# Local attention inside a fused kernel: one matmul for both heads' scores, one for both heads' values

## What is computed

```python
batch, n_heads, seq, head_dim = 4, 8, 576, 64          # factor = 4
q_d, k_d, v_d = means of q, k, v over groups of 4 positions   # 144 positions
out_d = softmax(q_d @ k_d.T / 8) @ v_d                  # each head
scores = q @ k.T / 8, kept where |i - j| < 4            # local band
out_local = softmax(scores) @ v
x = np.repeat(out_d, 4, axis=2) + out_local             # -> (2304, 512)
h = (x @ w1) * (x @ w2) @ w3;  x = h @ w_out            # d_ff = 1024
h = maximum(maximum(x @ u1, x @ u2), x @ u3);  y = h @ u_out   # d_ff = 768
```

## Time and profile before

| | |
|---|---|
| median of 3 runs | 726.11 us (725.23 to 726.6) |
| profiled execution | 725.54 us, span from first to last instruction 723.8 us |
| PE busy | 713.2 us, 99% |
| PE weight loads (beside matmuls) | 595.1 us, 82% |
| DVE / ACT / POOL busy | 219.8 / 193.0 / 210.9 us |
| granted TensorE clock | 1.00 |

### The profile page before, as it was taken

How to read it: one execution, slowest core, us unless ns; L and a number is a source line. 1 busy time by engine, 2 the same in 40 slices (tenths; PEclk the granted TensorE clock), 3 DMA queues, 4 the chain that set the end, 5 groups by cost and what they waited for, 6 DMA issues and landing times.

```text
span 723.8 us, 14645 instructions
## 1 busy us (share of the span) xinstructions
PE 713.2 (99%) x6560; PEld 595.1 (82%) x6560; DVE 219.8 (30%) x392; ACT 193.0 (27%) x417; POOL 210.9 (29%) x186
## 2 busy tenths in 40 slices
PE   6999999999999999999999999999999999999998
PEld 4778788888888888888888998888888888888898
DVE  3464554414453345411100455111111111111111
ACT  5465423322332233312221533111120112111110
POOL 5799423303232223321220231130122114011210
PEclk9999999999999999999999999999999999999999
DMA  9874122202221121122000320000001000000100
GB/s 321 264 233 142 53 74 74 74 24 75 74 75 54 54 92 58 40 80 81 1 1 0 117 73 1 1 35 24 1 0 60 1 0 25 34 1 1 43 16 29
DMA packets 18590, 43.57 MB, mean 60 GB/s; under 512 B 2144, under 2 KB 2912, under 8 KB 18528
## 3 DMA queue, kind: packets, MB, share of 16 engines
q1 hardware_dynamic: 18528, 42.64, 18.2%
HBM read 37.91 MB, written 4.72 MB: 59 GB/s over the span
## 4 chain that ended last, share of the span: by engine, by line
PE 97%; DMA 1%; POOL 1%; SPq 1%; ACT 0%; DVE 0%; issue 0%
PE psum L346 30%; PE psum L348 29%; PE psum L347 29%; PE psum L385 2%; PE psum L363 2%; PE psum L356 2%; PE psum L394 1%; PE psum L373 1%; DMA attention<-ident 1%; POOL weights_split L738 1%; SPq L310 0%; POOL acts_split L738 0%; ACT attention L622 0%; DVE psum L528 0%; DVE psum L533 0%
## 5 line engine op out<-in xcount | busy, mean ns | idle before, releaser
L346 PE MATMUL psum<-acts_split,weights_split 128*128 128x512 f32 (+1 forms) x992 | 370.3, 373 | 0.6 <-POOL weights_split L738 0.6
L348 PE MATMUL psum<-acts_split,weights_split 128*128 128x512 f32 (+1 forms) x992 | 366.0, 369 | 0.0
L347 PE MATMUL psum<-acts_split,weights_split 128*128 128x512 f32 (+1 forms) x992 | 365.8, 369 | 0.0
L346 PEld LDWEIGHTS psum<-acts_split,weights_split 128*128 128x128 f32 x992 | 187.0, 188 | 34.6 <-issue 2.6
L348 PEld LDWEIGHTS psum<-acts_split,weights_split 128*128 128x128 f32 x992 | 187.0, 189 | 31.7
L347 PEld LDWEIGHTS psum<-acts_split,weights_split 128*128 128x128 f32 x992 | 187.1, 189 | 30.1
L738 POOL TENSOR_TENSOR acts_split<-gate,acts_split 128x512 fp32r<-128x512 f32 (+1 forms) x70 | 82.5, 1179 | 438.0 <-ACT acts_split L622 438.0
L622 ACT ACTIVATE acts_split<-gate 128x512 fp32r<-128x512 f32 (+1 forms) x70 | 41.2, 589 | 246.9 <-DVE gate L608 152.0
L622 ACT ACTIVATE gate<-psum 128x512 f32<-128x512 f32 (+1 forms) x70 | 38.8, 555 | 130.3 <-PE psum L348 130.3
L738 POOL TENSOR_TENSOR acts_split<-xy,acts_split 128x512 fp32r<-128x512 f32 (+1 forms) x44 | 52.2, 1207 | 55.7 <-ACT acts_split L622 55.7
L582 DVE TENSOR_TENSOR gate<-gate,psum 128x512 f32<-128x512 f32 (+1 forms) x40 | 25.4, 634 | 129.0 <-PE psum L348 129.0
(11 more groups left out here) (42 smaller groups left out, 378.4 us busy)
## 6 DMA issues: line engine op xcount, KB each, us to landing
xy<-wa SPq DMA_DIRECT2D x40, 256.0 KB, 5.4
attention<-qk SPq DMA_DIRECT2D x16, 576.0 KB, 4.2
attention<-v_win SPq DMA_DIRECT2D x16, 384.0 KB, 3.4
attention<-wb SPq DMA_DIRECT2D x24, 256.0 KB, 3.0
attention<-v_down SPq DMA_DIRECT2D x16, 320.0 KB, 3.2
out_t<-attention SPq DMA_DIRECT2D x16, 256.0 KB, 2.0
out_t<-attention SPq DMA_DIRECT2D x4, 128.0 KB, 1.7
attention<-mask SPq DMA_DIRECT2D x1, 96.0 KB, 5.7
```

The lines of the kernel that those rows point to most:

```text
L346: pe.matmul(out, lhs[:, 0], rhs[:, 0], start=first, stop=False)
L347: pe.matmul(out, lhs[:, 0], rhs[:, 1], start=False, stop=False)
L348: return pe.matmul(out, lhs[:, 1], rhs[:, 0], start=False, stop=last)
```

## The change

1. The host lays k out twice, once for each head, with the other head's partitions set to zero. `load_qk` brings (128 x 3 x 576): q, k of head 0, k of head 1. `qk_sum` is three reductions: q on 128 partitions, and each head's k on its own 64.
2. A window's local scores of both heads are one matmul, 128 rows by 32 columns with 64 moving: 24 instead of 48. All go to bank 4.
3. The down-sampled scores are one tile of 128 rows a head (64 rows by 128 columns, into banks 5 and 6), and one with the last 64 rows of each (64 by 64, bank 7): four matmuls instead of six.
4. `prob` is dropped: the last product of the local softmax stays in PSUM, and the block transpose reads it there.
5. A window's local values of both heads are one matmul, 32 rows by 128 columns with 48 moving: 24 instead of 48. Each head's own half of the result is used, so `x_out` is two additions, of 64 partitions each.
6. `copy_turned` is two copies, which leave out the rows that two tiles share.

```diff
-        qk_sb = cut(2 * S).rearrange("p (a s) -> p a s", a=2)
+        qk_sb = cut(3 * S).rearrange("p (a s) -> p a s", a=3)
...
-                for j in range(DJ):
-                    for h in range(2):
-                        rows = slice(D * h, D * h + D)
-                        mm = pe.matmul(score_d[rows, j, :], qkd[rows, 0, DSTEP * j:DSTEP * j + DROWS], qkd[rows, 1, :],
-                                       start=True, stop=True)
+                heads = [slice(D * h, D * h + D) for h in range(2)]
+                for h, rows in enumerate(heads):
+                    pe.matmul(score_d[:, h, :], qkd[rows, 0, 0:P], qkd[rows, 1, :], start=True, stop=True)
+                for rows in heads:
+                    mm = pe.matmul(score_d[rows, 2, :], qkd[rows, 0, SD - DLAST:], qkd[rows, 1, :], start=True, stop=True)
                 mm.then_inc(down_scored, 1)
                 for t in range(TG * TI):
                     g, i = t // TI, t % TI
-                    for h in range(2):
-                        rows = slice(D * h, D * h + D)
-                        mm = pe.matmul(score_l[TW * i:TW * (i + 1), h, g, :], qk_sb[rows, 0, Q0[t]:Q0[t] + TW],
-                                       qk_sb[rows, 1, K0[t]:K0[t] + TW], start=True, stop=True)
+                    mm = pe.matmul(score_l[TW * i:TW * (i + 1), g, :, :], qk_sb[:, 0, Q0[t]:Q0[t] + TW],
+                                   qk_sb[:, 1:3, K0[t]:K0[t] + TW], start=True, stop=True)
...
-                    for h in range(2):
-                        mm = pe.matmul(bank(4 + i)[D * h:D * (h + 1), PV + TQ * g:PV + TQ * (g + 1)],
-                                       v_sb[rows, g, D * h:D * (h + 1)], prob_t[rows, h, g, own:own + TQ],
-                                       start=True, stop=True)
+                    mm = pe.matmul(bank(4 + i)[:, 2 * TQ * g:2 * TQ * (g + 1)], v_sb[rows, g, :],
+                                   prob_t[rows, g, :, own:own + TQ], start=True, stop=True)
...
-                dve.tensor_reduce(qkd, qk_sb.rearrange("p a (s j) -> p a s j", j=FACTOR), AX_X,
-                                  ALU.add).then_inc(qk_summed, 1)
+                four = qk_sb.rearrange("p a (s j) -> p a s j", j=FACTOR)
+                dve.tensor_reduce(qkd[:, 0, :], four[:, 0], AX_X, ALU.add)
+                dve.tensor_reduce(qkd[0:D, 1, :], four[0:D, 1], AX_X, ALU.add)
+                dve.tensor_reduce(qkd[D:P, 1, :], four[D:P, 2], AX_X, ALU.add).then_inc(qk_summed, 1)
...
-                dve.tensor_tensor(prob, score_l, lrc.unsqueeze(3).to_broadcast([P, 2, TG, TW]),
+                dve.tensor_tensor(score_l, score_l, lrc.unsqueeze(3).to_broadcast([P, TG, 2, TW]),
                                   ALU.mult).then_inc(local_scaled, 1)
                 dve.wait_ge(local_scaled, u + 1)
-                dve.transpose(prob_t.rearrange("p h g q -> p (h g q)"),
-                              prob.rearrange("p h g k -> p (h g k)")).then_inc(local_turned, 1)
+                dve.transpose(prob_t.rearrange("p g h q -> p (g h q)"),
+                              score_l.rearrange("p g h k -> p (g h k)")).then_inc(local_turned, 1)
...
-                dve.tensor_tensor(out, local, up, ALU.add).then_inc(x_ready, 1)
+                for h in range(2):
+                    rows = slice(D * h, D * (h + 1))
+                    add = dve.tensor_tensor(out[rows], local[rows, h],
+                                            up[rows].unsqueeze(4).to_broadcast([D, TG, TI, TQ // FACTOR, FACTOR]), ALU.add)
+                add.then_inc(x_ready, 1)
...
-                copy(prob_dt, turned_d).then_inc(turn_copied, 1)
+                copy(prob_dt[:, :, :, 0:P], turned_d[:, :, 0:2, :])
+                last = turned_d[:, :, 2, :].rearrange("p k (h q) -> p k h q", h=2)[:, :, :, DLAST - (SD - P):]
+                copy(prob_dt[:, :, :, P:SD], last).then_inc(turn_copied, 1)
...
-    qk = np.stack(turned, axis=2)
+    k_own = [np.where(np.arange(P)[:, None] // D == h, turned[1], np.float32(0)) for h in range(2)]
+    qk = np.stack([turned[0]] + k_own, axis=2)
```

More of the change, by code:

```diff
@@ L34 @@
 Q0 = [min(TQ * t, S - TW) for t in range(TG * TI)]
-DJ, DROWS, DSTEP, DOWN = 3, 64, 40, 48
+DJ, DLAST = 3, 64
 TD = SD // 2
@@ L200, in build @@
         vd = cut(2 * P, TD).rearrange("p (k c) -> p k c", k=2)
-        prob = cut(2 * TG * TW).rearrange("p (h g k) -> p h g k", h=2, g=TG)
-        prob_t = cut(2 * TG * TW).rearrange("p (h g q) -> p h g q", h=2, g=TG)
+        prob_t = cut(2 * TG * TW).rearrange("p (g h q) -> p g h q", g=TG, h=2)
         prob_d = cut(DJ * SD).rearrange("p (j k) -> p j k", j=DJ)
-        prob_dt_all = cut(2 * DJ * P + 88, TD)
-        prob_dt = prob_dt_all[:, 0:2 * DJ * P].rearrange("p (k c) -> p k c", k=2)
+        prob_dt = cut(2 * 2 * SD, TD).rearrange("p (k h q) -> p k h q", k=2, h=2)
         up_t = cut(SD)
@@ L210, in build @@
         dnb, dsum, drc = (cut(DJ) for _ in range(3))
[L211 to L221, removed]
+        lmax, lrc = (cut(2 * TG).rearrange("p (g h) -> p g h", h=2) for _ in range(2))
+        score_l = bank(4)[:, 0:2 * TG * TW].rearrange("p (g h k) -> p g h k", g=TG, h=2)
+        score_d = psum[:, 512 * 5:512 * 8].rearrange("p (j c) -> p j c", j=DJ)[:, :, 0:SD]
+        turned_d = psum[0:TD, 512 * 6:512 * 8].rearrange("p (k c) -> p k c", k=2)[:, :, 0:DJ * P].rearrange(
+            "p k (j q) -> p k j q", j=DJ)
+        PV = 2 * TG * TQ
+        pv_down = bank(5)[:, PV:PV + SD]
+        dmax, dsum_eps = (bank(6)[:, 432 + DJ * i:432 + DJ * (i + 1)] for i in range(2))
+        lsum, lsum_eps = (bank(4)[:, 480 + 2 * TG * i:480 + 2 * TG * (i + 1)].rearrange("p (g h) -> p g h", h=2)
                           for i in range(2))
@@ L372, in turns @@
                     for j in range(DJ):
-                        mm = pe.transpose(turned_d[:, kt, P * j:P * (j + 1)], prob_d[:, j, TD * kt:TD * (kt + 1)], ident)
+                        mm = pe.transpose(turned_d[:, kt, j, :], prob_d[:, j, TD * kt:TD * (kt + 1)], ident)
                 mm.then_inc(down_turned, 1)
@@ L391, in values @@
                     for h in range(2):
-                        first = DJ * P * kt + D * h
-                        own = prob_dt_all[:, first:first + 136 * DJ].rearrange("p (j c) -> p j c", j=DJ)[:, :, 0:DOWN]
-                        mm = pe.matmul(pv_down[D * h:D * (h + 1), :], vd[:, kt, D * h:D * (h + 1)], own,
+                        mm = pe.matmul(pv_down[D * h:D * (h + 1), :], vd[:, kt, D * h:D * (h + 1)], prob_dt[:, kt, h, :],
                                        start=kt == 0, stop=kt == 1)
@@ L565, in x_out @@
                 dve.wait_ge(up_ready, u + 1)
[L566 to L569, removed]
+                local = psum[:, 512 * 4:512 * 8].rearrange("p (i c) -> p i c", i=TI)[:, :, 0:PV].rearrange(
+                    "p i (g h s j) -> p h g i s j", g=TG, h=2, j=FACTOR)
+                up = up_t.rearrange("p (g i s) -> p g i s", g=TG, i=TI)
                 out = xy[:, T * p + S * b:T * p + S * (b + 1)].rearrange("p (g i s j) -> p g i s j", g=TG, i=TI, j=FACTOR)
-                dve.tensor_tensor(out, local, up, ALU.add).then_inc(x_ready, 1)
+                for h in range(2):
[3 more added lines that the diff above has]
+                add.then_inc(x_ready, 1)
             def product_low(i):
```

4 lines of the change are left out of this document (2 added, 2 removed).

## The result

The changed kernel is slower: 733.77 us median of 4 runs (732.84 to 735.1) against 725.67 for the kernel before (4 runs); the ratio is 1.0112, 95% interval 1.0089 to 1.0135. The profiled execution took 734.51 us with a span of 732.7, 8.9 more than the 723.8 of before.

What follows compares the result with a forecast made beforehand. PE's queue was taken as the bound. 6.1 - 3.3 + 0.9 + 0.9 + 0.6 + 0.4 + 0.5 = +6.1 us on the profiled 725.54 us gave 731.6 us, range 718 to 738.

Steps and rivals of the forecast that it cites:

- Local values: Local value matmuls on PE: the 128-column weight load sets the slot, 1.46 us against 1.08, +6.1 us for 16 units.
- (1): Start: the larger q and k load is first in the queue, so all behind it lands later, +0.9 us.
- (2): Before unit 1's scores: later landing, longer sum and doubled x_out make PE wait, +0.9 us.
- the rival of the count: Small matmuls on PE: the number of records binds, so values and scores get faster, 716 us; chance 0.20 in whole or part.
- Scores: Score matmuls on PE: down-sampled ones gain 0.04 us, local ones 0.18; -3.3 us for 15 units.
- (3): Before the scores of units 2 and 3: x_out ends later and there is little slack, +0.6 and +0.4 us.
- (4): After x_out of unit 3: an ACT copy, POOL's work and PE behind it come later, +0.5 us.
- the unchanged slot: Rival, local values: the slot stays 0.09 us, so no change, 725.5 us; chance 0.14.
- load and matmul in a row: Rival, local values: load and matmul of a tile never overlap, +13.1 us, 738.7; chance 0.12 with near cases.
- queued loads: Rival, local values: loads of the four row tiles queue, +4.2 us a unit, 792.9 us; chance 0.04.
- The waits of (2) to (4): Rival, start: these waits vanish because PE is late enough anyway, 729.2 us, inside the forecast's range.

Runs made afterwards that it cites:

- e1: Changed kernel with the local values again one matmul a head (48 instead of 24), x_out still two additions: 728.13 us, 1.0035 to the kernel before.
- e2: Changed kernel with 20 of the 24 local value matmuls of a unit moving 96 columns instead of 48, same weight loads: 734.11 us.
- e7: Changed kernel with each local score matmul of 64 moving columns cut into two of 32, same tile shape, 96 records a unit: 737.48 us.
- e4: Changed kernel with local values one matmul a head and x_out one addition, as before the change; scores stay merged: 724.87 us, 0.9987 to the kernel before.
- e5: Changed kernel with unit 1's scores at 18 instead of 15 in the table of visits and its turns at 23.5 instead of 22: 732.83 us.
- e6: e4 with q and k loaded small in two DMAs of 64 partitions, the other halves zeroed by DVE before unit 0: 726.32 us, 1.0015 to the kernel before.
- e9: Changed kernel with unit 0's q and k load large, bringing the zeros, and every later one two small DMAs of 288 KB: 734.25 us.

## Why the prediction came out as it did

731.6 us was forecast, 733.8 measured, on the right side and inside the range. The mechanism of the main term, local values bound by their loads, was right. What failed in the start are (1), a delay that didn't come, and the clock, which no term held; (1) cost the forecast little, because PE's earlier arrival only made the wait for the same landing (2) longer. Step by step:

- **Local values, +6.1 forecast, +6.4 measured.** 1.46 against 1.48 us. e1 and e2 show the mechanism: the loads of the four row tiles overlap, and each tile takes its next matmul 0.112 us later, the 0.11 of a load of 128 columns, with 48 or with 96 moving columns. By the Trainium skill (TensorE: Matmul & The Clock Gate, "LDWEIGHTS (loading the stationary operand)") I had estimated +0.34 a unit; the trace has +0.40 and agrees with the rule that rows don't count: 186 ns for 32 rows, 188 for 128. One argument of mine for it was wrong, though: I read the 0.090 against 0.079 us a slot in the kernel before as the load's doing. By e7 the count of records sets such a time, at 8.5 to 10 ns each on average. The count gave the old time and the load gives the new one; so the argument for the rival of the count was right about the kernel before.
- **Scores, -3.3 forecast, -2.8 measured.** The down-sampled ones came as worked out (0.45 and 0.39 against 0.446 and 0.392, averaged over visits); the local ones took 0.81 for 0.77: a slot of 64 moving columns is (0.81 - 0.13) / 12 = 0.057 us, not 0.053.
- **(1) Everything behind the larger first load 0.9 later: wrong, 0.06 measured.** The load itself landed 0.95 us later (5.26 for 4.31), and so did the first weights behind it (ACT copies them at 5.92 instead of 4.91). But the identity matrix's landing let DVE start at 11.83 instead of 11.78, although 295 KB more stood ahead of it. Bytes ahead divided by the mean rate don't give a landing here; issued at 5.15 in both kernels, it took 6.6 and 6.7 us. By 11.7 us 3.31 MB had been moved in either kernel, so the larger load had taken the place of other bytes, not of the identity matrix. Why it did, no run shows. That PE's later start goes into its old wait was right: 0.21 us of 1.12 are left.
- **(2) Wait before unit 1's scores, +0.9 forecast, 2.0 measured, and behind it 1.2 that no term held.** Landing, sum and additions were right to 0.3 us (23.56, 25.7 and 27.3). For the landing that may be luck: it was worked out from bytes ahead and a mean rate, as (1) was, and there this failed. PE was ready 0.8 us earlier than forecast, since (1) failed, so (1) and (2) together are 1.8 forecast against 2.1. What was missing is the clock: in two of the four executions, the profiled one among them, the wait of 2 us cost more than its length. Against the two at 1.000 (732.84 and 733.03) the forecast is 1.3 short.
- **(3) +0.6 and +0.4 forecast, 0.90 and 0.53 measured:** the mechanism was right, 0.4 short in all.
- **(4) +0.5 forecast, +0.8 measured, over another path.** Not the low part of x on POOL but the low part of a product on DVE (L505), which waits for ACT's copies, and these stand behind the copy of x on ACT. I had followed one of the two queues behind `x_out`.
- **Rivals.** The count of records, the unchanged slot and load and matmul in a row are out by 1.08 and 1.48 in e1 and e2; queued loads by the 1.48. The waits of (2) to (4) did not vanish.

In the profiled execution the start came out 2.0 us dearer than forecast (5.3 for 3.3), of which the clock is 1.2; the rest made 0.8 more (3.6 for 2.8).

## What to carry to other kernels

Before two small matmuls are merged, ask what sets the pace of each shape: the count of records, the moving columns, or the columns of the weight load. Halving the count helps down to the point where the wider tile's own load or movement takes over; here merging along the moving side gained 0.14 us a visit and merging along the stationary side lost 0.40. And look at what the merge asks of others: a larger load, a sum in three instructions and an addition in two stood on the stretch where PE waits for other engines, and together they cost 5.3 us in the profiled execution, beside 3.6 on PE itself. The second addition alone is 3.3 of the median (e1 against e4); the longer sum was never tried by itself.

## What the runs showed that I had not expected

- A wait of 2.04 us on PE was followed by granted clock 0.57 from 28 to 32 us; so were waits of 2.6 us (e1: 0.90 from 30 to 40 us) and 1.8 us (e5: 0.83). Waits of 1.39 us (e6), 1.30 us (e9) and 1.22 us (e4) were followed by a clock of 1.00. But these are single profiled executions. Of the same kernels, two in four executions of the changed one and three in five of e1 had a mean clock of 1.000, while three in four of e9 and two in twelve of e6 had 0.997 or 0.998. So the fall can differ from one execution of a kernel to the next, and the length of the wait alone isn't shown to decide it.
- A load of q and k with a third less data, in two DMAs, landed no earlier (23.49 against 23.56), while one issued 1.6 us earlier, ahead of four pieces of 256 KB, landed 4.9 us earlier.
- 96 records over four column tiles take 1.10 us and 48 with twice the columns 0.81: 96 small records need 8.5 to 10 ns each on average, also where tiles work side by side.
